# Expert layers by Strassen's seven block products, in three passes of 768 tokens

## The reference

```
attn_out = attention(q, k, v, tau)         # 4 batches, 8 heads, 576 positions, head size 64
                                           # scores below the row's maximum - tau are masked
x = attn_out as [2304 tokens, 512 features]
h = x @ moe_w_in                           # 512 -> 2048
x = (h - tanh(h)) @ moe_w_out              # 2048 -> 512
h = x @ moe2_w_in
out = (h * sigmoid(h)) @ moe2_w_out
```

## Time and profile before

| | |
|---|---|
| median of 3 runs | 1098.31 us (1098.05 to 1098.68) |
| the profiled execution | 1098.13 us, its span 1096.3 us |
| TensorE busy | 1076.1 us, 98% |
| VectorE, ScalarE, GpSimd busy | 557.6, 403.0, 267.3 us |
| attention, up to the first expert matmul | 297.6 us |
| granted clock of TensorE | 1.0 throughout |

### The profile page before, as it was taken

How to read it: one execution, slowest core, us unless ns; L and a number is a source line. 1 busy time by engine, 2 the same in 40 slices (tenths; PEclk the granted TensorE clock), 3 DMA queues, 4 the chain that set the end, 5 groups by cost and what they waited for, 6 DMA issues and landing times.

```text
span 1096.3 us, 15672 instructions
## 1 busy us (share of the span) xinstructions
PE 1076.1 (98%) x5808; PEld 870.7 (79%) x5808; DVE 557.6 (51%) x1341; ACT 403.0 (37%) x832; POOL 267.3 (24%) x243
## 2 busy tenths in 40 slices
PE   5999999999999999999999999999999999999998
PEld 5667767676688888888888889888888888888898
DVE  7999999999677543343343343622322222222222
ACT  6989888898732211121121111432211211111111
POOL 5767676676264100000000000544000000000000
PEclk9999999999999999999999999999999999999999
DMA  5213122230243200000000000342100100010010
GB/s 172 81 56 112 64 104 93 75 110 14 79 126 97 58 1 1 1 0 0 0 0 0 0 1 1 96 116 58 39 1 1 38 0 0 0 39 0 0 39 20
DMA packets 14939, 46.38 MB, mean 42 GB/s; under 512 B 1568, under 2 KB 2592, under 8 KB 14880
## 3 DMA queue, kind: packets, MB, share of 16 engines
q1 hardware_dynamic: 14592, 45.55, 12.8%
q10 hardware_dynamic: 288, 0.07, 0.0%
HBM read 40.89 MB, written 4.72 MB: 42 GB/s over the span
## 4 chain that ended last, share of the span: by engine, by line
PE 95%; DVE 1%; ACT 1%; POOL 0%; issue 0%; DVEq 0%; ACTq 0%
PE hid L797 36%; PE acc L813 36%; PE scores L754 9%; PE pv L717 8%; PE tps L776 6%; DVE x_lo L638 0%; ACT w_parts L481 0%; ACT x_hi L490 0%; DVE probs L615 0%; DVE probs L583 0%; ACT pT L432 0%; POOL q_parts L372 0%; DVE w_parts L668 0%; DVE stats L599 0%; ACT pR L434 0%
## 5 line engine op out<-in xcount | busy, mean ns | idle before, releaser
L797 PE MATMUL hid<-x_hi,w_parts 128*128 128x512 f32 (+1 forms) x1280 | 384.9, 368 | 3.2 <-DVE x_lo L638 2.1
L813 PE MATMUL acc<-g_hi,w_parts 128*128 128x512 f32 (+1 forms) x1280 | 384.1, 368 | 0.0
L797 PEld LDWEIGHTS hid<-x_hi,w_parts 128*128 128x128 f32 x1280 | 234.1, 189 | 44.8 <-DVE x_lo L638 2.2
L813 PEld LDWEIGHTS acc<-g_hi,w_parts 128*128 128x128 f32 x1280 | 234.2, 189 | 39.8
L797 PE MATMUL hid<-x_lo,w_parts 128*128 128x512 f32 (+1 forms) x640 | 235.4, 368 | 0.0
L813 PE MATMUL acc<-g_lo,w_parts 128*128 128x512 f32 (+1 forms) x640 | 235.4, 368 | 0.0
L652 DVE CAST g_hi<-h_act 128x512 fp32r<-128x512 f32 (+1 forms) x160 | 70.8, 443 | 270.4 <-ACT h_act L505 267.7
L396 POOL TENSOR_TENSOR w_parts<-w_raw,w_parts 128x1024 fp32r<-128x1024 f32 x30 | 73.3, 2448 | 400.3 <-ACT w_parts L481 400.3
L647 DVE TENSOR_TENSOR h_act<-hid,h_act 128x512 f32<-128x512 f32 (+1 forms) x80 | 51.0, 638 | 200.9 <-ACT h_act L502 200.9
L502 ACT ACTIVATE h_act<-hid 128x512 f32<-128x512 f32 (+1 forms) x80 | 44.4, 555 | 292.7 <-PE hid L797 292.7
L505 ACT ACTIVATE h_act<-hid 128x512 f32<-128x512 f32 (+1 forms) x80 | 44.4, 555 | 289.9 <-PE hid L797 289.9
(11 more groups left out here) (47 smaller groups left out, 768.2 us busy)
## 6 DMA issues: line engine op xcount, KB each, us to landing
w_raw<-w_in SPq DMA_DIRECT2D x32, 512.0 KB, 3.5
k_raw<-k_in SPq DMA_DIRECT2D x15, 576.0 KB, 4.1
q_raw<-q_in SPq DMA_DIRECT2D x15, 576.0 KB, 5.9
v_all<-v_in SPq DMA_DIRECT2D x16, 320.0 KB, 3.0
out<-xT SPq DMA_DIRECT2D x4, 1024.0 KB, 4.2
k_raw<-k_in SPq DMA_DIRECT2D x2, 288.0 KB, 3.4
out<-xT SPq DMA_DIRECT2D x1, 512.0 KB, 2.9
q_raw<-q_in SPq DMA_DIRECT2D x1, 224.0 KB, 4.2
```

What stands on the lines that cost most here:

```text
L797: last = pe.matmul(hid[f % HBANKS][:, 0:w], a, b[:, kc, 0:w], start=(kc == 0 and i == 0), stop=(kc == KC - 1 and i == 2))
L813: last = pe.matmul(acc[n][:, 0:w], a, b[f % GRING][:, 0:w], start=(f == 0 and i == 0), stop=(f == FT - 1 and i == 2))
```

## The change

Both matrices of an expert product are cut into 2 x 2 blocks, and Strassen's seven products of sums of blocks take the place of eight block products. Each product is still made of three part products. The tokens are taken in three passes of 768 per layer (two halves of `TW` = 384), so six passes `z`. In a pass, `hidden` has eight jobs `u` (FP = 8, each two tiles of hidden features): for each of the seven products 6 matmuls of 384 columns. `project` has 28 batches (7 products x 4), each 12 matmuls of 384 columns.

The results C11, C12, C21, C22 need each product in several places. Instead of adding complete products, the partial result is continued in PSUM: VectorE or ScalarE writes a seed, made from another bank, into a bank (`seed11`, `seed22`, `t5`, `c21_copy`, `diff`), and TensorE accumulates the next product on it with `start=False`.

The sums of blocks and their hi and lo parts are new work: for the first weight of a job on GpSimd (`w_sums_a`, `w_sums_b`), ScalarE (`w_hi_*`) and VectorE (`w_lo_*`) in each job of each pass, double-buffered; for the input once a pass (`x_sum`, `x_hi`, `x_lo`); for the hidden activations in each batch (`g_sum`, `g_hi`, `g_lo`).

The second weights' operands (7 products x 2 parts) are made once and kept in DRAM (`scr`), and streamed back for each batch, 512 KB each, into five slots `w2`. Layer 1's eight groups are made and stored during attention (`stage_piece`, `stage_hi_of`, `store_stage`, 1792 KB each), layer 2's in the jobs of passes 0 to 2 (`NEXT`; `load_next`, `next_sums_of`, `next_hi_of`, `next_lo_of`, `store_next`) through one buffer `stage_raw` and one `stage`. `product_of` makes the three part products of one product over both halves of the contraction. `seed22` and `difference` are written like `seed11`. `load_w2` waits for a free slot of five. The tokens' order in `xT` is changed so that a pass's halves are contiguous, and the host puts the output back in order.

```diff
+SPLITS = 3
+PASSES = LAYERS * SPLITS
+TW = TOKENS // SPLITS // 2
+WIDE = 2 * TW
+FP = DF // P // 2
+JOBS = PASSES * FP
...
+P_ORDER = (5, 4, 3, 1, 2, 7, 6)
+SUMMED = (4, 3, 1, 7, 6)
...
+NEXT = (0, 1, 2), (3, 4, 5), (6, 7)
...
+            def load_w(u):
+                m, j = u // FP // SPLITS, u % FP
+                if u < 2:
+                    sp.wait_ge(stage_sums, 5 * FP)
+                    sp.wait_ge(stage_lo, 4 * FP)
+                else:
+                    sp.wait_ge(w_sums, 4 * (u - 1))
+                    sp.wait_ge(w_split, 3 * (u - 2) + 1)
+                sp.dma_start(w_raw[u % 2][:].rearrange("p b c -> p (b c)"),
+                             w_in[:, 2 * FP * m + j]).then_inc(w_loaded[u % 2], 16)
+            def load_next(z, f):
+                if f == 0:
+                    sp.wait_ge(out_taken, 2 * PAIRS * BATCH)
+                else:
+                    sp.wait_ge(batch_done, BATCHES * z)
+                    sp.wait_ge(next_sums, 5 * f)
+                    sp.wait_ge(next_lo, 3 * (f - 1) + 1)
+                sp.dma_start(stage_raw[:].rearrange("p b c -> p (b c)"),
+                             w_in[:, 3 * FP + f]).then_inc(next_loaded, 16)
+            def store_next(f):
+                sp.wait_ge(next_lo, 3 * (f + 1))
+                sp.dma_start(scr[:, 1, :, f], stage[:].bitcast(F32)
+                             .rearrange("p s a c -> p s (a c)")).then_inc(next_stored, 16)
...
+            for z in range(PASSES):
+                nexts = NEXT[z] if z < len(NEXT) else ()
+                for j in range(FP):
+                    if j % 2 == 0 and j // 2 < len(nexts):
+                        load_next(z, nexts[j // 2])
+                    if j == 1:
+                        for i in range(W2_SLOTS):
+                            load_w2(BATCHES * z + i)
+                    if j < FP - 1 and FP * z + j + 4 < JOBS:
+                        load_w(FP * z + j + 4)
+                    if j % 2 == 1 and j // 2 < len(nexts):
+                        store_next(nexts[j // 2])
+                for i in range(W2_SLOTS, BATCHES):
+                    load_w2(BATCHES * z + i)
+                    if i == 9 and FP * z + FP + 3 < JOBS:
+                        load_w(FP * z + FP + 3)
...
+            def w_sums_a(u):
+                raw, sums = w_raw[u % 2], w_sum[u % 2]
+                pool.wait_ge(w_loaded[u % 2], 16 * (u // 2 + 1))
+                if u < 2:
+                    pool.wait_ge(stage_stored, 16 * FP)
+                else:
+                    pool.wait_ge(m1_done, u - 1)
+                pool.tensor_tensor(sums[:, 2, 1], raw[:, 0], raw[:, 3], ALU.add).then_inc(w_sums, 1)
+                pool.tensor_tensor(sums[:, 3:5, 1], raw[:, 0:4:2], raw[:, 1:4:2], ALU.add).then_inc(w_sums, 1)
+            def w_sums_b(u):
+                raw, sums = w_raw[u % 2], w_sum[u % 2]
+                if u >= 2:
+                    pool.wait_ge(m7_done, u - 1)
+                pool.tensor_tensor(sums[:, 5, 1], raw[:, 2], raw[:, 0], ALU.subtract).then_inc(w_sums, 1)
+                pool.tensor_tensor(sums[:, 6, 1], raw[:, 1], raw[:, 3], ALU.subtract).then_inc(w_sums, 1)
+            def next_sums_of(f):
+                pool.wait_ge(next_loaded, 16 * (f + 1))
+                if f > 0:
+                    pool.wait_ge(next_stored, 16 * f)
+                for i, (a, b, how) in enumerate(W_SUMS):
+                    pool.tensor_tensor(stage[:, 2 + i, 1].bitcast(F32), stage_raw[:, a], stage_raw[:, b],
+                                       how).then_inc(next_sums, 1)
...
+            for u in range(2):
+                w_sums_a(u)
+                w_sums_b(u)
+            for z in range(PASSES):
+                nexts = NEXT[z] if z < len(NEXT) else ()
+                for j in range(FP):
+                    u = FP * z + j + 2
+                    if u < JOBS:
+                        w_sums_a(u)
+                    if j % 2 == 0 and j // 2 < len(nexts):
+                        next_sums_of(nexts[j // 2])
+                    if u < JOBS:
+                        w_sums_b(u)
...
+            def w_hi_raw(u):
+                act.wait_ge(w_loaded[u % 2], 16 * (u // 2 + 1))
+                if u < 2:
+                    act.wait_ge(stage_stored, 16 * FP)
+                else:
+                    act.wait_ge(m1_done, u - 1)
+                act.activation(w_op[u % 2][:, 0:2, 0], w_raw[u % 2][:, 0:4:3], ACT.Copy).then_inc(w_hi, 1)
+            def w_hi_a(u):
+                act.wait_ge(w_sums, 4 * u + 2)
+                act.activation(w_op[u % 2][:, 2:5, 0], w_sum[u % 2][:, 2:5, 1], ACT.Copy).then_inc(w_hi, 1)
+            def w_hi_b(u):
+                act.wait_ge(w_sums, 4 * u + 4)
+                act.activation(w_op[u % 2][:, 5:7, 0], w_sum[u % 2][:, 5:7, 1], ACT.Copy).then_inc(w_hi, 1)
...
+            def take_t5(u):
+                act.wait_ge(m5_done, u + 1)
+                if u > 0:
+                    act.wait_ge(seed11_done, u)
+                if u % FP == 0 and u > 0:
+                    act.wait_ge(p_seed11_done, 2 * (u // FP))
+                act.activation(t5[:], bank[u % 2]["12"], ACT.Copy).then_inc(t5_taken, 1)
...
+            def hidden(z):
+                take_t5(FP * z)
+                for j in range(FP):
+                    u = FP * z + j
+                    if 2 <= u + 1 < JOBS:
+                        w_hi_b(u + 1)
+                    if u + 2 < JOBS:
+                        w_hi_raw(u + 2)
+                    if j + 1 < FP:
+                        take_t5(u + 1)
+                    if j == 0:
+                        take_c21(u)
+                        nonlinear("21", u)
+                        nonlinear("12", u)
+                    if u + 2 < JOBS:
+                        w_hi_a(u + 2)
+                    if j == FP - 2:
+                        g_hi_of(BATCHES * z)
+                    if z < len(NEXT) and j % 2 == 1 and j // 2 < len(NEXT[z]):
+                        next_hi_of(NEXT[z][j // 2])
+                    nonlinear("22", u)
+                    nonlinear("11", u)
+                    if j + 1 < FP:
+                        take_c21(u + 1)
+                        nonlinear("21", u + 1)
+                        nonlinear("12", u + 1)
+                for i in range(1, 3):
+                    g_hi_of(BATCHES * z + i)
...
+            def next_lo_of(f):
+                dve.wait_ge(next_hi, 3 * f + 1)
+                dve.tensor_tensor(stage[:, 0:2, 1], stage_raw[:, 0:4:3], stage[:, 0:2, 0].bitcast(F32),
+                                  ALU.subtract).then_inc(next_lo, 1)
+                for i, s in enumerate((slice(2, 5), slice(5, 7))):
+                    dve.wait_ge(next_hi, 3 * f + 2 + i)
+                    dve.tensor_tensor(stage[:, s, 1], stage[:, s, 1].bitcast(F32), stage[:, s, 0].bitcast(F32),
+                                      ALU.subtract).then_inc(next_lo, 1)
...
+            def seed11(u):
+                z, j = divmod(u, FP)
+                dve.wait_ge(t5_taken, u + 1)
+                dve.wait_ge(m4_done, u + 1)
+                if j >= 2:
+                    dve.wait_ge(c_done, 4 * (u - 2) + C_POS["11"] + 1)
+                elif z > 0:
+                    dve.wait_ge(y_by_act, 6 * (z - 1) + 5 + j)
+                dve.tensor_tensor(bank[j % 2]["11"], bank[j % 2]["21"], t5[:], ALU.subtract).then_inc(seed11_done, 1)
...
+            def hidden(z):
+                seed11(FP * z)
+                for j in range(FP):
+                    u = FP * z + j
+                    if 2 <= u + 1 < JOBS:
+                        w_lo_b(u + 1)
+                    if j + 1 < FP:
+                        seed11(u + 1)
+                    if j == 0:
+                        gate("21", u)
+                        difference(u)
+                        seed22(u)
+                        gate("12", u)
+                    if u + 2 < JOBS:
+                        w_lo_raw(u + 2)
+                    gate("22", u)
+                    if u + 2 < JOBS:
+                        w_lo_a(u + 2)
+                    gate("11", u)
+                    if j == FP - 2:
+                        g_lo_of(BATCHES * z)
+                    if z < len(NEXT) and j % 2 == 1 and j // 2 < len(NEXT[z]):
+                        next_lo_of(NEXT[z][j // 2])
+                    if j + 1 < FP:
+                        gate("21", u + 1)
+                        difference(u + 1)
+                        seed22(u + 1)
+                        gate("12", u + 1)
+                g_lo_of(BATCHES * z + 1)
...
+            def project(z):
+                for i in range(BATCHES):
+                    if i + 3 < BATCHES:
+                        g_sum_of(BATCHES * z + i + 3)
+                    if i + 2 < BATCHES:
+                        g_lo_of(BATCHES * z + i + 2)
...
+            steps(BATCH - 1, range(STEPS, TAIL), False)
+            for z in range(PASSES):
+                u0 = FP * z
+                m5(u0)
+                m4(u0)
```

(17 more changed lines are left out.)

769 lines of the change are left out of this document (547 added, 222 removed).

## The result

The changed kernel takes 1133.4 us in the median of 4 runs (1132.4 to 1135.9) against 1098.5 beside it: a ratio of 1.0316, with a 95% interval of 1.0304 to 1.0328. The direction was the forecast one; 1103 and the range up to 1128 were not. The profiled execution spans 1132.3 us, 36.0 more than before, where the sum said 4.9 more.

What follows compares the result with a forecast made beforehand. TensorE, busy 98%, was taken as the bound. Terms -89.8 - 2.0 + 12.0 + 23.4 + 53 + 3 + 5 + 0.3 = +4.9 took the 1096.3 us span to 1101, timed 1103; range 1060 to 1128.

Steps and rivals of the forecast that it cites:

- the matmuls: Expert part: 4032 matmuls of 384 columns at 173.3 ns, 698.8 us, saving 89.8 us.
- the starts: Start of each pass: TensorE waits 1.8 us before m2 of the second job, six times; +12.0 us in all.
- the way into the projection: Hidden part to projection: waits of 2.6 us before batch 1, 2.3 or 0.3 before batch 0; +23.4 us.
- rival 2: Layer 1's jobs: port waits make VectorE the bound, up to 1.1 us in 16 plain jobs, 1120 us; chance 0.10.
- Rival 4: Projection: the weight stream starves it, 239 us more if only one load in flight counted; chance 0.02.
- the staging: Making layer 2's second-weight operands in layer 1's jobs: 9 us for first groups, 44 for five later ones; +53 us.
- rival 1: Layer 2's staging hides, its term falling from 53 to 5, about 1055 us; chance 0.12, half-way (1075 to 1092) 0.22.
- rival 3: TensorE's clock falls after the staged jobs' 5 us stalls, perhaps 20 us in all, 1123 us; chance 0.09.
- I take +3: Attention: staging pieces on GpSimd and ScalarE delay some exponentials and one load; 3 us, bounds 0 and 10.
- +5: Hand-over from attention to the expert part: late last-pair output and queued roundings add 5 us, bounds 2 and 9.
- the old stalls: Layer switch: the earlier kernel's waits of 0.31 and 1.74 us for `x_lo` go, saving 2.0 us.
- the mark that the prediction set for being wrong: One stated sign of a wrong account: the hand-over starts beyond 310 us.

Runs made afterwards that it cites:

- e2: Changed kernel without the staging of layer 2's second weights; layer 2 reads layer 1's second weights instead: 1075.9 us against the changed kernel's 1133.4.
- e13: Changed kernel with layer 2's staging spread: two groups in each of passes 0 to 3, in pieces over several jobs, second group begun later: 1093.3 us.
- e1: Changed kernel plus 365 matmuls whose results nobody reads, put just ahead of TensorE's known waits: 1126.0 us.
- e8: Kernel without layer 2's staging (1075.9 us), plus unread matmuls in the short waits at pass starts, before the projection and before its second batch: 1065.5 us.
- e3: Changed kernel with attention staging only two of layer 1's eight groups, the other batches reading those two: 1129.3 us.
- e16: Changed kernel with attention's staging allowed from its eighth step instead of its third, all eight groups still made: 1133.8 us.
- e12: Changed kernel with ScalarE's last four input roundings and first job's last weight sums' rounding moved behind the last attention copies: 1133.8 us.
- e14: Changed kernel with the last four layer inputs placed behind the last attention copies and the second job's weights, on ScalarE and VectorE: 1131.2 us.

## Why the prediction was wrong

**Right: the matmuls, the starts, the way into the projection.** 282 matmuls in 49.15 us are the 173.3 ns of the sum and 0.28 at the end. The waits are 1.76 us at the starts (1.8 forecast), 2.4 to 2.5 before batch 1 (2.6), 2.7, 2.7 and 2.1 before batch 0 in layer 1 (2.3), 0.24 in layer 2 (0.3). VectorE's port did not make it the bound: rival 2 falls with e2, where all jobs of layer 1 are plain and the 282 matmuls behind each start run without a wait. Rival 4 falls too: no wait for weights anywhere in the changed kernel.

**Right as a time: the staging.** The cycle was 22.9 us in the mean of five (23.3), the first group's `seed22` wait 3.2 (2.2, and 0.7 for `w_lo_a`). From the first group's wait to the last one's, 350.06 to 395.38 in pass 0, go 45.3 us for 168 matmuls that take 29.1 at full pace: 8.1 a group, and 8.7 and 8.3 in the other two passes, where the sum had 8.8. That is 42 for five groups and 10.5 for the three first ones, 52.4 for a term of 53. But it is not all waiting, as the term had it: some 15 of it is TensorE at slow pace. e2's 57.6 is a wider measure, since it also holds changes of pace elsewhere. That the staging could be hidden was rival 1; it was not in this order, but e13 shows that 40 us of it can be.

**Wrong, first: the pace behind a wait, which the sum put at nothing.** The reason was one row: "Against: the stall of 1.74 us at 697.9 was followed by the full pace". One stall that kept its clock was taken for a rule, and rival 3 got 0.09. From the first product's matmul at 320.1 to 1128.8, behind the issue of the last, TensorE takes 808.7 us where the sum has 787.2. They are made up of 698.8 of matmuls at full pace, 68 of waits, 8 of ends (0.28 us at each of 29 stops) and, as what is left, some 33 of slow pace. The waits with their ends, 76, are 12 less than the 12.0 + 23.4 + 53 of the sum; the 33 stand in no term of it.

In the staged jobs the slow pace fills time that would be waited out: that is the 15 us above, and e1 with its clock of 0.989 has the groups no closer. At the starts of passes and at the projection it comes on top: 2.2 to 2.3 us behind each 1.76 us start of passes 0 to 2, 1.6 in pass 3, 1.6 behind batch 0 in passes 1 and 2 and none in pass 0, 0.7 behind each wait of 2.5 before batch 1 in layer 1 and 1.5 behind those of 2.4 in layer 2. That is about 18.5 of the 21.5; the other 3 are the waits before the projection, 26 with their ends for 23.4. e8 shows 10.4 us of such pace by itself. Rival 3's price of 20, 1123 for the whole, comes near by luck: it put the cost behind the 5 us stalls of the staged jobs, where it added next to nothing, and not behind the short waits. The Trainium skill, "TensorE: Matmul & The Clock Gate", Part 1, names the idle TensorE's return to the low clock; this case's runs agree, and what one wait costs comes from the rows.

**Wrong, second: "I take +3" and "+5" for attention and hand-over.** Together they were to bring the first expert product to about 309.0 (301.0 before, counted as the span less the expert matmuls, the old stalls and the end); it came at 320.1, so 19.1 for 8. The last pair's values are loaded at 269.6 instead of 258.0, which puts 11.6 of it in attention and 7.5 in the hand-over. In attention 6.7 us come in the first 54, where ScalarE stands 4.5 us before the first staged load with the first exponentials behind it, and 3.6 near 216 (the load of values there is at 216.3; in e3, with two groups for eight, it is at 212.4). The sum had counted the staging's busy time in a steady pair and not its queue at the start. But e16 shows that the 6.7 can be moved and not saved; what sets them stays open. In the tail the second context half waited 4.9 us where the sum had 3, and its 16 matmuls then took 4.11 us where 2.16 is the full pace (e12): the hand-over too has slow pace that no term held. e12 and e14 show that undoing this wait frees little or nothing. The expert part started beyond 310, the mark that the prediction set for being wrong.

**The account.** +21.5 in the expert part, +11.1 in attention and hand-over, and 1.5 less behind the last matmul's issue (3.5 us for 5.0) make the 31.1 between 1101.2 and 1132.3. The expert part is the larger piece, and most of it is pace.

## What to carry to other kernels

Price a wait on TensorE as the wait and the slow pace behind it (here nothing to 2.7 us for waits of 1.8 to 5.2), and don't let one stall without a penalty stand for all. Work in line costs by the longest thing it waits for, not by its busy time: the same groups cost 57.6 us with a round of store and load in every second job, and some 17 when a pass had two groups for three and each was cut in pieces over two or three jobs. Order the queues by what the bound engine wants next, and test such edits together as well as alone: here single orders did between 5 us of harm and 13 of good, the spread staging gave 40, and all together 74.

## What was not expected of the hardware

A wait of 1.76 us was enough for the clock to fall, but not always: the same wait at the start of a pass cost 2.2 to 2.3 us of pace in passes 0 to 2, 1.6 in pass 3 and nothing in passes 4 and 5 (49.15 us for 282 matmuls behind 891.30), as the one of 1.74 in the kernel before cost nothing. In e2, whose layer 2 differs only in where its second weights are read from, it cost nothing in pass 4 and 1.6 in pass 5:

```profile
830.84 49.17 PE L1314 MATMUL b<-x_op,w_op 128*128 128x384 f32 x282 [1.76 <-DVE b L1073]
...
954.58 50.73 PE L1314 MATMUL b<-x_op,w_op 128*128 128x384 f32 x282 [1.76 <-DVE b L1073]
```

So the place in the program alone doesn't decide. No run here tells what does. And filling idle waits with matmuls that nobody reads made a kernel 1.0% faster (e8 against e2) with nothing else changed.
